# Two moves in the order of transfers: layer 0's padding rows stored four tiles later, and the third part of a weight image stored five chunks earlier

## What is computed

```python
def _moe_ref(x, w_gate, w1, w2):
    logits = x @ w_gate
    expert_idx = np.argmax(logits, axis=1)
    ...                       # gate_w: softmax probability of the chosen expert
    for e in range(E):
        mask = expert_idx == e
        h = np.maximum(x[mask] @ w1[e], 0.0)
        out[mask] = gate_w[mask, None] * (h @ w2[e])
```

## Time and profile before

| | us |
|---|---|
| median of 3 runs | 1282.5 |
| lowest and highest of them | 1275.85, 1284.53 |
| the profiled execution | 1281.93 |
| its span in the trace | 1280.4 |
| TensorE busy in it | 1161.9 (91%) |
| DVE, ACT, POOL busy | 855.9, 615.3, 436.3 |

### The profile page before, as it was taken

One profiled execution on the slowest core, in us unless ns is written; L12 is line 12 of the kernel. 1 busy time (PEld: TensorE's weight loads), 2 busy tenths in 40 slices (PEclk: granted clock), 3 DMA queues, 4 the chain that ended last, 5 costly groups with the idle time before them and its releaser, 6 DMA issues.

```text
span 1280.4 us, 38886 instructions
## 1 busy us (share of the span) xinstructions
PE 1161.9 (91%) x13470; PEld 1054.3 (82%) x13470; DVE 855.9 (67%) x2335; ACT 615.3 (48%) x1083; POOL 436.3 (34%) x478
## 2 busy tenths in 40 slices
PE   2578774999889999999999999999999999999996
PEld 2567763888779888889999989888999998999996
DVE  2899997879889999997777787733333443334332
ACT  1777775345456555554545445333333333333332
POOL 1077786633323433432222222322222221222222
PEclk9776685999999999999999999999999999999999
DMA  8588966799997799566443426476424546424451
GB/s 222 176 279 283 296 216 201 177 204 232 255 289 172 189 288 280 144 207 168 107 112 94 119 67 153 94 193 179 117 57 113 165 112 167 114 55 109 112 136 56
DMA packets 236048, 214.78 MB, mean 168 GB/s; under 512 B 176895, under 2 KB 209307, under 8 KB 229954
## 3 DMA queue, kind: packets, MB, share of 16 engines
q1 hardware_dynamic: 209408, 148.85, 44.7%
q0 software_dynamic: 25520, 64.49, 17.1%
q10 hardware_dynamic: 1042, 0.47, 0.2%
HBM read 114.22 MB, written 69.62 MB: 144 GB/s over the span
## 4 chain that ended last, share of the span: by engine, by line
PE 56%; DVE 22%; issue 7%; DMA 6%; SPq 4%; ACT 3%; DVEq 0%; POOL 0%; ACTq 0%; POOLq 0%
PE bank L871 55%; DVE am L1136 3%; DVE hl L1367 2%; DMA wslot<-image 2%; DVE split L1211 2%; PE bank L876 1%; DMA stage<-in_moe_w 1%; SPq L426 1%; DVE split L1214 1%; DVE wslot L1238 1%; DVE wam L1100 1%; DVE wam L1098 1%; SPq L427 1%; DVE xsl L1140 1%; ACT rowt L727 1%
## 5 line engine op out<-in xcount | busy, mean ns | idle before, releaser
L1367 DVE SCALAR_TENSOR_TENSOR hl<-bank,hh 128x512 f16<-128x512 f32 x480 | 331.1, 690 | 336.3 <-ACT hh L812 330.4
L812 ACT ACTIVATE hh<-bank 128x512 f16<-128x512 f32 x480 | 286.3, 596 | 461.3 <-PE bank L871 452.1
L871 PE MATMUL bank<-xT,wslot 128*128 128x256 f16 (+1 forms) x3920 | 467.3, 274 | 13.4 <-DMA xT<-rows 7.5
L871 PE MATMUL bank<-wslot,hh 128*128 128x192 f16 x3136 | 421.5, 247 | 8.5 <-DVE hl L1367 4.9
L871 PEld LDWEIGHTS bank<-xT,wslot 128*128 128x128 f16 (+1 forms) x3920 | 328.7, 98 | 70.9 <-issue 22.3
L871 PE MATMUL bank<-wslot,hl 128*128 128x192 f16 x1568 | 386.3, 246 | 0.0
L871 PEld LDWEIGHTS bank<-wslot,hh 128*128 128x128 f16 x3136 | 279.4, 98 | 28.6 <-issue 13.5
L699 POOL DMA_INDIRECT out_tokens<-y,idxt x120 | 116.7, 972 | 364.7 <-ACT y L824 311.4
L640 POOL DMA_INDIRECT rows<-rowt,idxp x120 | 126.4, 1053 | 321.5 <-PE bank L871 196.7
L871 PEld LDWEIGHTS bank<-wslot,hl 128*128 128x128 f16 x1568 | 153.6, 98 | 0.1
L615 POOL DMA_INDIRECT rows<-rowab,idxa x96 | 107.4, 1119 | 55.1 <-issue 39.7
(11 more groups left out here) (175 smaller groups left out, 1270.8 us busy)
## 6 DMA issues: line engine op xcount, KB each, us to landing
wslot<-image SPq DMA_DIRECT2D x21, 1024.0 KB
split<-image SPq DMA_DIRECT2D x16, 1024.0 KB
wslot<-image SPq DMA_DIRECT2D x21, 768.0 KB, 5.2
split<-image SPq DMA_DIRECT2D x16, 768.0 KB, 4.9
image<-split POOLq DMA_DIRECT2D x18, 512.0 KB
image<-split SPq DMA_DIRECT2D x8, 1024.0 KB, 4.2
image<-split POOLq DMA_DIRECT2D x9, 768.0 KB
stage<-in_moe_w SPq DMA_DIRECT2D x8, 768.0 KB, 9.8
```

The lines of the kernel that those rows point to most:

```text
L812: nc.scalar.activation(hh[:, c, :], bank[c][:, :], ACT.Relu).then_inc(hh_out, 1)
L871: return nc.tensor.matmul(o, a, b_, start=start, stop=stop, skip_group_check=True)
L1367: V.scalar_tensor_tensor(hl[:, c, :], bank[c][:, :], 0.0, hh[:, c, :], ALU.max, ALU.subtract).then_inc(hl_out, 1)
```

## The change

The pads of layer 0 are stored after the loads of tiles 12, 13, 14 and 15, and the wait for the scatters stands ahead of all of them. On POOL, the third part of the image is stored right after the row scatter of chunk 5, ahead of the first part, and its wait for chunk 10 goes. What is stored and loaded, and by which queue, stays the same.

```diff
             with sp.Fori(1, 2) as i:
                 quad(loads, i, False, 0, False)
+            sp.wait_ge(table_ready, 3)
+            for g in range(8, 12):
+                one(loads, g)
             sp.wait_ge(pads_ready, 1)
-            sp.wait_ge(table_ready, 3)
+            for i in range(2 * SLOTS):
+                sp.wait_ge(scat_a[i], 8 * G * len(range(i // 2, STEPS, SLOTS)))
             for c in range(E // 2):
-                one(loads, 8 + c)
+                one(loads, 12 + c)
                 for e in (2 * c, 2 * c + 1):
                     store_pad(sp, 0, e)
-            for i in range(2 * SLOTS):
-                sp.wait_ge(scat_a[i], 8 * G * len(range(i // 2, STEPS, SLOTS)))
-            for g in range(12, 4 * MIXQ):
-                one(loads, g)
             sp.wait_ge(pads_stored, 16 * E)
...
                 next_weights(i, 2)
                 scatter_row(i * 2 - 2, 0, 1)
+                next_image(i, 2)
                 paced(i * (4 * NP) + 6)
                 next_image(i, 0)
...
                 scatter_row(i * 2 - 2, 0, 3)
-                paced(i * (4 * NP) + 10)
-                next_image(i, 2)
                 scatter_pair(i * 2 - 1, 1)
```

## The result

The changed kernel is slower by half a per cent: median 1285.6 us of 20 runs against 1279.0 us of 20 runs of the kernel before, ratio 1.0047 with a 95% interval of 1.0027 to 1.0068, so about +6 us. My sum of the terms was +1.5 us. Single runs of either kernel scatter by 15 to 19 us, and the execution that was profiled after the change took 1294.6 us, 9 us over its median. The page: TensorE's busy time and its clock (compare).

What follows compares the result with a forecast made beforehand. Bound: TensorE gaps in layer 0's quads 1 to 3 (four tiles each), 14.0 us extra with DMA engines 92% busy or more. Terms +0.3 - 2.0 + 2.3 + 0.7 + 0.2 = +1.5 us on 1281.9, written 1283.5; range 1275 to 1292.

Steps and rivals of the forecast that it cites:

- Quad 2: Layer 0, tiles 8 to 11: ACT gains 1.8 us, TensorE's gap falls from 4.1 to 2.3 us; -2.0 us.
- the price of 0.79 MB: Third part queued ahead of the first two on POOL: costs 2.0 us alone, 5.8 us sharing with SP's queue.
- Quad 3: Layer 0, tiles 12 to 15: pads' data delay tile 15's w1; +2.3 us, between +1.3 and +4.0.
- Quad 4: Layer 0, tiles 16 to 19: SP's wait for all pads delays tile 18's rows and ids; +0.7 us.
- Quads 4 to 8, the third part: Layer 0, tiles 16 to 35: image parts still land in time for L746; +0.2 us, between 0 and 5.
- Quad 1: Layer 0, tiles 4 to 7: late w2 gap stays, parts up to 1 us late; +0.3 us, -0.5 to +1.
- The late parts: ACT before L746, quads 1 to 8: first two parts 5.8 us late each; +9.7 us, 1291.6; chance 0.13.
- The pads rival: Quad 3 +4, tile 18 late by 2 us, no gain in quad 2; about +6 us, 1288; chance 0.12.
- The stalls: Rival: all three stalls, in quads 1 to 3, go as less is in flight; -14 us, 1268; chance 0.04.
- the signs that I had named: L746 wait 1 to 4 us in quad 2, quads 5, 6, 8 at 36.1; wrong if quad 1 changes over 2.

Runs made afterwards that it cites:

- the third part alone: Only the image's third part moved from chunk 10 to chunk 5, pads left after tiles 8 to 11, against the kernel before: ratio 1.0024.
- The pads-only kernel: Only the pads moved, to after tiles 12 to 15, third part left at chunk 10, against the kernel before: ratio 1.0050.
- the second trace: Each kernel traced again unchanged: the changed kernel at ratio 1.0054 to the kernel before; the kernel before in one run, with no ratio.
- The kernel without a last pair: Changed kernel with pads stored three, three and two after tiles 12 to 14, none after tile 15: ratio 1.0006 to the kernel before.

## Why the prediction was right and where it was not

The time (1285.6) lies in the range of 1275 to 1292 and on the side of zero that I gave. Much of that is luck. The forecast of 1283.5 stood on three runs of the kernel before with a median of 1282.5, which is 1279.0 over 20 runs; this 3.5 us hides most of the distance between my +1.5 us and the measured +6. And of the five terms four came out beyond their own ranges (quads 1 to 4), one of them (quad 2) downwards against three upwards, so that the net stayed in the range. Step by step, with the means over the two traces of each kernel:

**Quad 2: forecast -2.0 us (0 to -5.2), measured -5.7.** The mechanism was right: the first two image parts still make ACT wait a little (0.98 and 1.63 us; forecast 2.6), the third no longer does, and the gap falls from 4.14 and 6.56 to 0.61 and 0.75 us. Mis-sized was the price of 0.79 MB ahead of the first two parts. I took the two parts 0.9 us late; in the changed traces L746's counterpart starts 23.2 (328.76 - 305.61) and 23.8 us after the quad's first raw load, in those before 23.9 (326.58 - 302.71) and 23.2, so on the mean they were not late at all. With the third part alone moved it starts at 24.6 us: the 0.79 MB cost about 1.1 us, in one trace, where I had 2.0 to 5.8. The other part of the difference is that the kernel before is worse here than its first trace showed (43.9 us in the second). The pads-only kernel gives what belongs to the pads: 38.5 us; the third part alone: 37.7 us.

**Quad 3: forecast +2.3 us, measured +4.3.** I named tile 15's w1, and it is there: its gap went from 2.42 to 2.88 and 3.68 us, and two earlier gaps of 1.55 and 1.62 us (1.61 and 1.07 in the second trace), also ended by weight loads, stand besides. I argued that the load's issue did not matter, because it sat in a backlogged queue. In the changed trace SP issues it only here:

```profile
358.76 1.99 SPq L371 DMA_DIRECT2D rows<-padrow  x2
362.49 0.35 SPq L445 DMA_DIRECT2D wslot<-image  x1
```

That is 20.7 us after the quad's first raw load (341.78), where it was 15.2 us (358.40 - 343.21), and it was used 28.8 us after it against 26.5. So the load was issued 5.5 us later and used some 8.1 us after its issue, where it took 11.21 before to land. My term has the right size for this load, 2.3 us, and the wrong reason: I had put the later issue at nothing and the landing at 13 to 14 us. The other gaps I did not have in the sum. In all but one of the kernels that shortened quad 2, quad 3 came out at 43.0 to 48.3 us, six of them with no pads there. Only the third part alone (39.7) escapes. That quad 2's saving is largely given back in quad 3, because both wait for the same backlog of transfers, fits these traces, but I only argue it: no run changed the loads themselves, and what ends the gaps in quad 3 differs from kernel to kernel (a weight load of SP's, the raw w2, or an image part). How much of quad 3's +4.3 us is the pads there and how much this backlog stays open. In the sum over quads 2 and 3 the kernel before has 81.4 and 82.7 us, the change 80.2 and 81.1.

**Quad 4: forecast +0.7 us (0 to 2), measured +4.6. This is the step that failed by most.** The mechanism was named (SP held at the wait, tile 18's second half and its ids late), the price was too low by a factor of more than six. I put the pads' landing near 385.5 and the ids 4.7 us later than before, landing in 7.36 us, 1.4 us too late. In the changed trace, counted from POOL's first transfer of the quad, the ids go out at 9.8 us (395.59 - 385.76) where it was 4.3 (388.31 - 384.06): 5.6 us later. And the rows ahead of them take 9.15 us to land, not 7.4. POOL's queue was busy beside them in the way told below for quad 6: from 400.0 to 403.4 us it moved 276 packets with 1.18 MB, SP's queue 270 packets with 0.03 MB. Together the DVE reads the ids 4.1 us late. The clock adds to it: 0.61 over the 3.4 us behind the gap (403.80 to 407.20), 1.3 us. I had also let the forecast for this place shrink to the half of what I had worked out, on the ground that a shorter landing would save it. In the second trace the same later issue (9.5 us into the quad) met a landing of 6.48 us, the ids were 1.5 us late, and the next tile's wait of 2.13 us made up the rest. The kernel without a last pair (quad 4 at 36.9 and 0.5% faster) shows that nearly all of this term belongs to the two pads ahead of the wait.

**Quads 4 to 8, the third part: forecast +0.2 us, measured +2.1 in quad 6 alone.** I asked only whether ACT would find the parts landed, and it did (the longest wait is 0.24 us). I did not ask what SP loads at that time. SP's w1 load in quad 6 is issued where it was before (14.3 us into the quad, against 14.6), but POOL's queue still has a backlog then. The load took 11.05 us and stopped TensorE for 2.80 us (1.52 in the second trace). The trace shows how the two queues share the engines. From 1.0 to 5.0 us after the issue (packets, MB, share of the engines; the changed kernel, then the one before):

```profile
q0 software_dynamic: 359, 1.38, 92.4%
q1 hardware_dynamic: 358, 0.09, 10.4%
...
q1 hardware_dynamic: 115, 0.79, 53.5%
q0 software_dynamic: 183, 0.58, 50.3%
```

In the changed kernel each queue moved one packet for each of the other's, but POOL's packets held 3.8 KB and SP's 0.25 KB. The w1 load's own packets are of 8 KB (48 in 1 us, 0.39 MB, from 485.00), so the small ones are of what SP issued ahead of it, transposed rows (471.44 and 472.90). The w1 data stood behind small packets that advanced one for one with POOL's large ones; before, POOL's queue ran dry about 3 us after the issue. The same stretch of the other traces goes with it: SP moved 0.08 to 0.18 MB in the other four of chunk 5, 0.33 to 0.44 in the four of chunk 8, and 0.45 to 1.01 in the other four of chunk 10. The five traces with chunk 5 have 37.0 to 39.8 us there, the four with chunk 8 have 36.4 to 37.0.

**Quad 1: forecast +0.3, measured +1.6,** within what its traces scatter.

**The rivals.** The late parts (0.13) are not what happened: ACT waits nowhere as that case has it, and the load that came late was SP's. The Trainium skill ("DMA: Bandwidth & Descriptors", "Queues, rings and completion order") has each DMA engine go round robin between queue rows, packet by packet. The trace agrees in quad 6, with 359 packets against 358. What I concluded from it does not hold: an equal share of packets was 1.38 MB against 0.09, so SP's backlogged row did not keep its share of the bytes. The pads rival (0.12), "quad 3 +4 and tile 18 late", is the nearest to what came: about its +6, by more in quad 4 and with a gain in quad 2 that it did not have. The stalls did not vanish. Of the signs that I had named, quad 6 did not stay at 36.1 us, L746's counterpart waits there (0.24 us in one trace, nothing in the other), and the w1 load ahead of tile 15 did not take 13 to 14 us. Quad 1 changed by over 2 us in the first trace and by 1.6 on the mean.

## What to carry to other kernels

When a store is moved to a later place in a queue, look at the wait that follows it: its price is the issue and the landing of the last store, and it is paid by everything queued behind the wait, here the rows of a tile two tiles ahead. Where one engine's stores are pulled forward, ask of every other queue what it loads in that stretch, not only who waits for the stores, and look at packets as well as bytes: here a queue of 0.25 KB packets beside one of 3.8 KB packets got a fifteenth of the bytes. And where several stretches in a row are bound by the same transfers, a stall removed in one may come back in the next, so count it only over the sum of them (argued here, not shown). Of the kernels tried, the third part at chunk 8 alone and the pads after tiles 1 and 2 are the fastest (0.9971 and 0.9972, upper ends of the intervals just under 1).

## What the hardware showed that I had not expected

The clock does not follow from the length of a gap alone. I had taken a gap of 2.4 us or more to cost 1.7 us of half clock and left open what lies between 1.4 and 2.4. Layer 1 has a gap of 2.15 us (2.16 in one) at the same place in all four traces of the two kernels. In the kernel before, TensorE's row and the window behind it:

```profile
753.19 0.51 PE L876 MATMUL bank<-ident,rowt 128*128 128x128 f16 x6 [2.15 <-DVE rowt L1145]
```

```profile
753.50:757.00 3.50, 3.50 (x56) 3.31 (x55) 1.57 (x5) 2.22 (x3) 0.00 (x0) 1.00 0.02 5
```

and in the changed one:

```profile
761.56 0.82 PE L875 MATMUL bank<-ident,rowt 128*128 128x128 f16 x6 [2.15 <-DVE rowt L1144]
```

```profile
761.80:765.20 3.40, 3.40 (x25) 2.85 (x23) 1.08 (x2) 1.41 (x2) 0.00 (x0) 0.55 0.00 0
```

The granted clock stayed at full speed (2.4 GHz) in one and fell to about half (1.2 GHz) for most of 3.4 us in the other, some 1.5 us of work for the same gap. In both TensorE had worked without a pause and at full clock before the gap (all of 745 to 749 and of 753.5 to 757.5 us). Nor does it belong to the kernel, for in the second traces it is the other way round (the kernel before, then the changed one; their clocks behind the gap are 0.52 over 3.4 us and 1.00):

```profile
748.98 0.82 PE L876 MATMUL bank<-ident,rowt 128*128 128x128 f16 x6 [2.16 <-DVE rowt L1145]
...
752.00 0.51 PE L875 MATMUL bank<-ident,rowt 128*128 128x128 f16 x6 [2.15 <-DVE rowt L1144]
```

That can be a part of why single executions scatter by 15 us, though no run here singles it out. It is a reason not to read the profiled execution of the changed kernel, 9 us over its median, alone.
